# Eight subtractions of the first weight matrix move from VectorE to GpSimd

## What is computed

```
f = lb + (1 - lb) * sigmoid(f_logit)
h = f[:, t] * h + (1 - f[:, t]) * x[:, t]      # y[:, t] = h
a = y @ w_in                                   # 256 -> 2048
g = where(a >= 1, a, where(a <= -1, 0, (a + 1)**2 / 4))
out = g @ w_out                                # 2048 -> 256
```

## Time and profile before

| | |
|---|---|
| time, median of 3 runs | 1022.43 us (1022.42 to 1022.43) |
| time of the profiled execution | 1022.77 us |
| its span | 1021.0 us |
| PE busy | 998.4 us (98%), 4376 matmuls |
| DVE busy | 884.9 us (87%) |
| ACT busy | 885.2 us (87%) |
| POOL busy | 0.2 us, 4 instructions |
| granted TensorE clock, mean | 0.989 of full |

### The profile page before, as it was taken

The page is one execution under the profiler, slowest core; times in us unless marked ns, Lnnn a source line. Parts: engine busy times, 40 slices in busy tenths (PEclk is TensorE's granted clock), DMA queues, the critical chain, the costliest instruction groups (busy, mean ns, idle before and its releaser), DMA issues.

```text
span 1021.0 us, 12955 instructions
## 1 busy us (share of the span) xinstructions
PE 998.4 (98%) x4376; PEld 818.9 (80%) x4376; DVE 884.9 (87%) x1327; ACT 885.2 (87%) x1562; POOL 0.2 (0%) x4
## 2 busy tenths in 40 slices
PE   7788999999999999999999999999999999999998
PEld 3567788888888888888888888888888888888887
DVE  7899898898888888989888889889888898988775
ACT  5788988998998998898898899899899889888886
POOL 0000000000000000000000000000000000000000
PEclk8799999999999999999999999999999999999999
DMA  5200210210110120020021021011012002000100
GB/s 204 101 21 0 83 39 1 83 42 1 47 78 1 41 83 1 5 89 32 1 83 41 1 83 43 1 52 74 1 42 83 0 12 84 25 1 1 42 1 39
DMA packets 13282, 42.38 MB, mean 42 GB/s; under 512 B 1440, under 2 KB 2464, under 8 KB 13216
## 3 DMA queue, kind: packets, MB, share of 16 engines
q1 hardware_dynamic: 13072, 41.56, 12.0%
q10 hardware_dynamic: 144, 0.00, 0.0%
HBM read 29.10 MB, written 12.45 MB: 41 GB/s over the span
## 4 chain that ended last, share of the span: by engine, by line
PE 89%; DVE 5%; ACT 3%; issue 1%; DMA 1%; SPq 0%; DVEq 0%; ACTq 0%
PE acc L684 16%; PE acc L686 16%; PE acc L685 16%; PE chain L684 8%; PE chain L686 8%; PE chain L685 8%; PE cross L686 4%; PE cross L685 4%; PE cross L684 4%; PE side L685 2%; PE side L686 2%; PE side L684 2%; DVE h L527 1%; DMA gate<-f_logit_chunks 1%; ACT g L292 1%
## 5 line engine op out<-in xcount | busy, mean ns | idle before, releaser
L684 PE MATMUL acc<-g_hi,w_out_lo 128*128 128x512 f32 (+1 forms) x768 | 297.9, 388 | 0.0
L685 PE MATMUL acc<-g_lo,w_out_hi 128*128 128x512 f32 (+1 forms) x768 | 297.7, 388 | 0.0
L686 PE MATMUL acc<-g_hi,w_out_hi 128*128 128x512 f32 (+1 forms) x768 | 297.7, 388 | 0.0
L313 ACT CAST g_hi<-g 128x512 fp32r<-128x512 f32 (+1 forms) x384 | 235.6, 613 | 40.0 <-DVE g L548 34.7
L560 DVE TENSOR_TENSOR g_lo<-g,g_hi 128x512 fp32r<-128x512 f32 (+1 forms) x384 | 261.9, 682 | 8.7
L306 ACT ACTIVATE g<-g 128x512 f32<-128x512 f32 (+1 forms) x384 | 240.6, 627 | 3.1
L548 DVE SCALAR_TENSOR_TENSOR g<-g,h 128x512 f32<-128x512 f32 (+1 forms) x288 | 196.6, 683 | 48.2 <-ACT g L306 44.9
L292 ACT ACTIVATE g<-h 128x512 f32<-128x512 f32 (+1 forms) x288 | 177.2, 628 | 41.1 <-DVE h L527 38.4
L527 DVE TENSOR_TENSOR h<-part,cross 128x512 f32<-128x512 f32 (+1 forms) x192 | 130.4, 679 | 52.5 <-ACT part L287 51.2
L684 PEld LDWEIGHTS acc<-g_hi,w_out_lo 128*128 128x128 f32 x768 | 144.4, 188 | 29.2 <-issue 0.4
L685 PEld LDWEIGHTS acc<-g_lo,w_out_hi 128*128 128x128 f32 x768 | 144.4, 188 | 28.8
(11 more groups left out here) (56 smaller groups left out, 930.2 us busy)
## 6 DMA issues: line engine op xcount, KB each, us to landing
y<-x_chunks SPq DMA_DIRECT2D x20, 512.0 KB, 4.2
gate<-f_logit_chunks SPq DMA_DIRECT2D x20, 512.0 KB, 4.1
out_chunks<-result SPq DMA_DIRECT2D x10, 1024.0 KB, 4.3
w_in_f<-w_in_pairs SPq DMA_DIRECT2D x8, 256.0 KB, 6.5
w_out_f<-w_out_pairs SPq DMA_DIRECT2D x8, 256.0 KB, 4.3
gate<-f_logit_chunks SPq DMA_DIRECT2D x4, 240.0 KB, 4.6
y<-x_chunks SPq DMA_DIRECT2D x4, 240.0 KB, 4.7
out_chunks<-result SPq DMA_DIRECT2D x1, 960.0 KB, 5.4
```

Of the source, the lines that this page charges most:

```text
L313: nc.scalar.copy(g_hi[:, t, 0:cols], g[:, t, 0:cols]).then_inc(g_hi_ready[t], 1)
L684: nc.tensor.matmul(dst, w_lo, v_hi, start=start, stop=False, skip_group_check=more)
L685: nc.tensor.matmul(dst, w_hi, v_lo, start=False, stop=False, skip_group_check=more)
L686: return nc.tensor.matmul(dst, w_hi, v_hi, start=False, stop=stop, skip_group_check=more)
```

## The change

The eight instructions `in_low(0)` to `in_low(7)` are issued by GpSimd, one behind the other, each with the wait for `in_high(j)` that it had; they are taken out of VectorE's order. Everything else keeps its place. VectorE gets one wait for all eight before `even_low(1)`, in window 6 of the first span, because that instruction writes over `w_in_f`.

```diff
+        @block.gpsimd
+        def _(pool):
+            def in_low(j):
+                pool.wait_ge(w_in_hi_ready, j + 1)
+                nc.gpsimd.tensor_tensor(w_in_lo[:, j], w_in_f[:, j], w_in_hi[:, j].bitcast(f32),
+                                        ALU.subtract).then_inc(w_in_lo_ready, 1)
+
+            for j in range(PAIRS):
+                in_low(j)
...
         @block.vector
...
-            def in_low(j):
-                dve.wait_ge(w_in_hi_ready, j + 1)
-                nc.vector.tensor_tensor(w_in_lo[:, j], w_in_f[:, j], w_in_hi[:, j].bitcast(f32),
-                                        ALU.subtract).then_inc(w_in_lo_ready, 1)
...
             def even_low(q, ks=slice(0, KT)):
                 cols, s = width(q), q % 2
+                if q == 1:
+                    dve.wait_ge(w_in_lo_ready, PAIRS)
...
                 if q == 0:
                     out_low(j)
-                    if j + 2 < PAIRS:
-                        in_low(j + 2)
...
             scan(0, 1, 1)
-            in_low(0)
             t2(0)
...
             save(0)
-            in_low(1)
```

## The result

The changed kernel takes 1029.77 us (median of 6, 1029.48 to 1030.85) against 1022.42 us (6 runs, 1022.25 to 1022.55): ratio 1.0074, 95% interval 1.0061 to 1.0087, which is 7.35 us slower. The forecast was 1030.6 us, with 1025.5 to 1035 for its own range. The profiled execution took 1029.66 us with a span of 1027.9 us.

The account below looks back on a forecast made before the run. VectorE's order was taken to bound the first span's windows. Windows +5.2 us and start +3.0 us gave +8.2 us on 1022.43 us: 1030.6 us, its own range 1025.5 to 1035, the overall range 1014.5 to 1034.5.

Parts of the forecast that it names:

- The bound: First span's windows: VectorE's order is the bound; each tenth added or removed reaches the kernel's end, up to TensorE's slack.
- GpSimd's length: Each in_low on GpSimd takes 2.0 us, against 1.09 us on VectorE.
- VectorE's stand: VectorE beside each GpSimd instruction: bounds 0 and 2.0 us; the upper end was taken.
- VectorE first: Rival: GpSimd gets in only when VectorE reads PSUM or waits; sum −2.5, 1020 us; chance 0.12.
- No interference: Rival: VectorE runs freely beside GpSimd; sum −7.5, 1015.0 us; chance 0.23.
- shared by element: Rival: both engines go on, VectorE slower by about what it saved; within ±1.5 us, 1022.4 us; chance 0.12.
- The windows: Six windows of the first span: VectorE held 2.0 us, less the work removed; 0.87 us each, +5.2 us.
- The start: Before the windows: t2(0) later by 1.05 us, odd_low(0) and save(0) by 2.0 us; together +3.0 us.
- The sign named for the second: Start, profile after: save(0) at about 26.5 us; at about 24.6 or earlier, the start's second term is wrong.
- The clock: TensorE may fall to half clock in two or three more windows; 8 slower matmuls cost 1.5 us, some inside slack.

Follow-up runs that it names:

- the windows alone: Changed kernel with in_low(0) and in_low(1) given back to VectorE, GpSimd subtracting only pairs 2 to 7: 1027.53 us.
- the same trick: Changed kernel with one more wait on GpSimd, so that in_low(1) begins only when save(0) is done: 1028.56 us.
- the two placements beside the PSUM instructions: Changed kernel, pairs 0 and 1 on VectorE, GpSimd's others begun when the instruction ahead of add_h11, or add_h11 itself, is done: 1015.23 and 1018.79 us.
- the start alone: Changed kernel with pairs 2 to 7 given back to VectorE, GpSimd subtracting only pairs 0 and 1: 1025.23 us.

## Why the prediction was right

**The bound.** VectorE's order set the windows of the first span: taking the subtraction out, with the stand laid into a wait, brought 1.22 us in the window shown. What left VectorE is a little more than the 1.16 us of the sum. From `out_low` to `activated` it was 1.85 us before (44.95 to 46.80) and is 0.61 here (53.77 to 54.38), so 1.24 us: the wait listed as 0.15 us was 0.23 by start-to-start distances.

**GpSimd's length** was taken as 2.0 us. It is 2.12 us beside the PSUM instructions, the cleanest case. The 2.36 to 2.66 us in the changed kernel include its own wait for VectorE's running instruction: counted from that one's end, the eight are 1.89 to 1.99 us (at 49.01 us, 2.45 less the 0.46 to the end of `activated`). The estimate of 1.97 us worked out from the Trainium skill (GPSIMD Engine Reference, section on elementwise cycle accounting) is 7% under the 2.12.

**VectorE's stand.** Both ends were open, 0 and 2.0 us; 1.94 us was measured for the `sums`. The two-input form and the small copy are held, the forms with a PSUM operand are not. The rival "VectorE first" fails: GpSimd gets in after whichever instruction is running, though VectorE's follow each other without a gap. "No interference" and "shared by element" fail with the same lines; the instructions behind and ahead of the stretched one keep their lengths.

**The windows** were priced at +5.2 us. `add_h11` is late by 2.87, 3.95, 4.63, 5.31, 6.19 and 6.87 us in the second to the seventh window, after 2.02 at the gate's arrival. So they cost 4.85 us (12.45 us for a window where 12.7 was foretold); the run with the windows alone gives 5.26, with a clock that fell more often. Singly they are 0.85, 1.08, 0.68, 0.68, 0.88 and 0.68. The +0.87 of the sum was right for two of them only, those in which 1.0 to 1.04 us was taken out. In the other four the 1.24 us above left VectorE, and 1.93 less 1.24 is the 0.68 measured; the 1.08 is such a window with 0.4 us of the clock on top. VectorE's order alone thus costs 4.45 us and not 5.2.

**The start** was priced at +3.05 us: 2.7 by the distance from the last `scan`, 2.96 by the experiment. Of the 2.7, `t2(0)` gives 0.85 (1.05 in the sum) and `save(0)` 1.9 (2.0 in the sum). The sign named for the second, `save(0)` at about 26.5 us, holds for its end (25.80 in an execution that is 0.6 us ahead) and not for its start (23.74), since the stand lies inside it. The step was not exact: GpSimd did not get in ahead of `odd_low(0)`. The two began within 0.01 us (23.16 and 23.17), `odd_low(0)` went first and kept its 0.65 us, and only `save(0)` stood. As both lead to the same transfers, the sum hardly changed.

**The clock** was left out of the sum and put into the range. It did fall once more than in the kernel before, in the 40s, behind a gap of 2.91 us; the low stretch in the 90s has its counterpart before, at 88 us. The fall in the 40s cost about 0.4 us: that window's 1.08 against the others' 0.68. The prediction had 1.5 us for a fall before slack.

The sum of the two measured parts, 2.7 + 4.85 = 7.55 us, meets the medians' 7.35. The forecast of 8.2 is 0.85 us above the medians. The mechanism and the two places where it costs are as foretold; that the total is so near is in part luck, as terms that were 0.75 and 0.3 us too high met a fall of the clock of 0.4 us that the sum did not have.

One rival's sum is off: the terms of "no interference" add to 7.65 us and not 7.5, which changes nothing here.

**What was missed.** The forecast saw GpSimd beside the PSUM instructions only as a rival's accident, worth −2.5 us. As a placement it is worth −7.0, since the half microsecond still standing falls into a wait for ScalarE that the gap list shows as 0.29 us and the start-to-start distances as 0.5.

## What to carry to other kernels

An idle GpSimd is not free help for a busy VectorE: an instruction that reads SBUF stops VectorE's next instruction with two SBUF inputs, or a copy, for about its own reading time, here 1.94 us to save 1.0 to 1.25. Start it so that it runs beside VectorE instructions with a PSUM operand, and let what is left over fall on an instruction whose successor waits anyway, once the timeline shows that nothing else hangs on it: ahead of `add_h11(0)` the same trick gave 1.1 us instead of 1.9. Look for the cost in the length of VectorE's instructions: no wait is listed for it.

## What the runs showed of the hardware

- A VectorE copy of 128x2 is held as long as a large instruction: 2.06 us instead of 0.16. What it releases, here SyncE's queue, is held with it.
- GpSimd's subtraction takes 2.12 us for 896 elements a partition when nobody is in its way, 2.4 ns an element, twice VectorE's 1.09 us. Its memset of 640 takes 0.63 us, held nobody and was held by nobody.
- After the start, TensorE's granted clock fell to half (1.2 of 2.4 GHz) in no place in two variants (the two placements beside the PSUM instructions), in one place in the kernel before, and in three in the windows alone. Each fall stood behind a gap of 1.38 us or more (1.38 us in the windows alone, 2.04 in the start alone, 2.91 in the changed kernel). The gap alone does not decide it: behind 1.69 us at 86.12 us it fell in the kernel before, behind 1.68 us at 88.48 us in the start alone it did not. By `add_h11`, a fall cost 0.2 us (that of the kernel before: its window takes 12.03 us, and 11.86 in the start alone without it) to 0.5 us of a window. None of the runs isolates it.
